# A sparse-attention plus feed-forward kernel: the first queries in a transfer of their own, and half of three up groups of block 0 moved into the round ahead

## What is computed

```python
scores = scale * np.matmul(q, k.transpose(0, 1, 3, 2))
kth = np.partition(scores, -top_k, axis=-1)[..., -top_k:-top_k + 1]
scores = np.where(scores >= kth, scores, -1000000000.0)
...
x = attn_out.transpose(0, 2, 1, 3).reshape(2304, 512)
h = x @ w_in
g = h * np.tanh(np.where(h > 20.0, h, np.log1p(np.exp(np.minimum(h, 20.0)))))
y = g @ w_out
```

## Time and profile before

| | |
|---|---|
| median of three runs | 761.02 us |
| the profiled execution: its time | 761.13 us |
| its span, first to last instruction | 759.3 us |
| PE busy | 720.5 us (95%) |
| DVE busy | 700.5 us (92%) |
| ACT busy | 570.3 us (75%) |
| POOL busy | 494.3 us (65%) |

### The profile page before, as it was taken

How to read it: one execution, slowest core, us unless ns; L and a number is a source line. 1 busy time by engine, 2 the same in 40 slices (tenths; PEclk the granted TensorE clock), 3 DMA queues, 4 the chain that set the end, 5 groups by cost and what they waited for, 6 DMA issues and landing times.

```text
span 759.3 us, 16003 instructions
## 1 busy us (share of the span) xinstructions
PE 720.5 (95%) x6056; PEld 625.3 (82%) x6056; DVE 700.5 (92%) x1512; ACT 570.3 (75%) x942; POOL 494.3 (65%) x590
## 2 busy tenths in 40 slices
PE   4258999999999999999999999999999999999998
PEld 2147888888989898979898989898888888888987
DVE  5999999999999999999999999999999999999600
ACT  3576978787879787878787777878796969687831
POOL 1877858576766666666667585848585858585813
PEclk9998999999999999999999999999999999999999
DMA  7560000031230000111110000001122000000000
GB/s 273 179 214 14 8 22 8 22 104 57 66 102 9 12 20 8 40 33 38 47 52 8 23 8 22 9 22 43 57 78 91 6 22 8 22 2 15 1 15 15
DMA packets 22684, 34.06 MB, mean 45 GB/s; under 512 B 2384, under 2 KB 11600, under 8 KB 22096
## 3 DMA queue, kind: packets, MB, share of 16 engines
q1 hardware_dynamic: 22608, 33.04, 13.3%
HBM read 28.31 MB, written 4.72 MB: 43 GB/s over the span
## 4 chain that ended last, share of the span: by engine, by line
PE 92%; DVE 6%; DMA 0%; issue 0%; ACT 0%; POOL 0%; SPq 0%
PE ps_u L397 35%; PE ps_y L412 27%; PE ps_o L379 10%; PE ps_s L351 9%; PE ps_s L332 9%; DVE left L601 3%; DVE top L607 2%; PE ps_o L372 1%; PE ps_s L328 1%; DVE top L592 1%; DMA q_sb<-q_in 0%; POOL p_sb L674 0%; ACT x_sb L459 0%; ACT xT L499 0%; ACT y_sb L528 0%
## 5 line engine op out<-in xcount | busy, mean ns | idle before, releaser
L607 DVE MAX8 top<-left 128x8 f32<-128x576 f32 x432 | 304.8, 747 | 0.0
L397 PEld LDWEIGHTS ps_u<-xT,win 128*128 128x128 f32 x2304 | 262.5, 192 | 13.8 <-issue 11.1
L397 PE MATMUL ps_u<-xT,win 128*128 128x128 f32 x2304 | 271.8, 277 | 0.7 <-ACT xT L499 0.7
L601 DVE MATCH_REPLACE8 left<-top,left 128x576 f32<-128x576 f32 x288 | 211.8, 743 | 0.0
L659 POOL TENSOR_TENSOR p_sb<-x_sb,p_sb 128x576 f32<-128x576 f32 x144 | 202.4, 1422 | 8.5 <-ACT p_sb L469 8.4
L489 ACT ACTIVATE pT<-ps_s 128x512 f32<-128x512 f32 (+1 forms) x144 | 85.6, 646 | 71.1 <-PE ps_s L351 71.1
L478 ACT ACTIVATE p_sb<-p_sb,neg_max 128x576 f32<-128x576 f32 x144 | 110.6, 769 | 27.7 <-POOL p_sb L659 27.2
L674 POOL TENSOR_SCALAR p_sb<-p_sb,recip 128x576 f32<-128x576 f32 x144 | 106.2, 747 | 35.6 <-DVE recip L582 35.6
L412 PE MATMUL ps_y<-w_hi,g_hi 128*128 128x512 f32 x288 | 117.9, 409 | 0.0
L469 ACT ACTIVATE p_sb<-x_sb,limit 128x576 f32<-128x576 f32 x144 | 105.5, 772 | 12.6 <-POOL limit L649 12.5
L412 PE MATMUL ps_y<-w_hi,g_lo 128*128 128x512 f32 x288 | 112.5, 391 | 0.0
(11 more groups left out here) (30 smaller groups left out, 603.5 us busy)
## 6 DMA issues: line engine op xcount, KB each, us to landing
v_sb<-v_in SPq DMA_DIRECT2D x32, 320.0 KB, 3.5
k_sb<-k_in SPq DMA_DIRECT2D x16, 288.0 KB, 3.3
q_sb<-q_in SPq DMA_DIRECT2D x68, 64.0 KB, 1.8
g_raw<-w_out SPq DMA_DIRECT2D x8, 512.0 KB, 4.4
win<-w_in SPq DMA_DIRECT2D x4, 1024.0 KB, 8.9
y_out<-y_sb SPq DMA_DIRECT2D x16, 256.0 KB, 2.0
y_out<-y_sb SPq DMA_DIRECT2D x4, 128.0 KB, 2.3
q_sb<-q_in SPq DMA_DIRECT2D x1, 256.0 KB, 3.4
```

The costliest lines, as they stand in the source:

```text
L397: mm = pe.matmul(ps_u[:, n % 2, i, :], win[:, k, P * f:P * f + P], xT[:, k, :], start=(k == 0), stop=(k == KC - 1), skip_group_check=True)
L601: dve.match_replace(out=left[:, t, :], in_to_replace=best[:, t, EIGHT * r:EIGHT * r + EIGHT], in_values=x[t] if r == 0 else left[:, t, :], ...
L607: dve.max(best[:, t, EIGHT * r + EIGHT:EIGHT * r + 2 * EIGHT], left[:, t, :]).then_inc(found, 1)
```

## The change

The queries of duo 0 get a transfer of their own (64 KB) ahead of the keys of pair 0; those of duos 1 to 3 follow behind the keys. `copy_xT(0)` is cut in two: `copy_xT_early` copies the pairs 0 and 1 of `ps_o` as soon as `values(1)` is through, in the round of -1, and `copy_xT(0)` the other two. On PE `up_begin(j)` runs the eight matmuls with k = 0 and 1 of the groups j = 0, 1 and 2 in the round of -1, and `up(0, j)` the eight with k = 2 and 3. Group 2 stands in the bank of `ps_y` for this block. The four loads of `w_in` have a semaphore each.

```diff
+EARLY, BEGUN = 2, 3
...
-                sp.dma_start(win[:, k, :], w_in[P * k:P * k + P, :]).then_inc(win_loaded, 16)
+                sp.dma_start(win[:, k, :], w_in[P * k:P * k + P, :]).then_inc(win_loaded[k], 16)
...
+            sp.dma_start(q_sb[:, 0, :], q_in[0, :, :]).then_inc(q_loaded[0], 16)
             load_k(0)
-            sp.dma_start(q_sb[:, :, :], q_in[0:QS, :, :].rearrange("s p c -> p s c")).then_inc(q_first, 16)
+            sp.dma_start(q_sb[:, 1:QS, :], q_in[1:QS, :, :].rearrange("s p c -> p s c")).then_inc(q_first, 16)
...
             def values(s):
...
+                if s == 2:
+                    pe.wait_ge(xT_begun, 1)
...
+            def up_bank(m, j):
+                if m == 0 and j == 2:
+                    return ps_y[:, :].rearrange("p (i c) -> p i c", i=FPG)
+                return ps_u[:, (GROUPS * m + j) % 2, :, :]
+
+            def up_begin(j):
+                if j == 0:
+                    pe.wait_ge(win_loaded[0], 16)
+                    pe.wait_ge(win_loaded[1], 16)
+                    pe.wait_ge(xT_begun, 1)
+                for i in range(FPG):
+                    f = FPG * j + i
+                    for k in range(EARLY):
+                        pe.matmul(up_bank(0, j)[:, i, :], win[:, k, P * f:P * f + P], xT[:, k, :],
+                                  start=(i == 0 and k == 0), stop=False, skip_group_check=True)
...
             def up(m, j):
...
-                if n >= 2:
+                if n >= 3:
                     pe.wait_ge(up_copied, n - 1)
+                begun = m == 0 and j < BEGUN
...
-                    for k in range(KC):
+                    for k in range(EARLY if begun else 0, KC):
...
             def down(m, j):
...
                 if m == 0 and j == 0:
                     pe.wait_ge(wlo_ready, WCHUNKS)
+                    pe.wait_ge(up_copied, BEGUN)
...
                 values(4 * m + 4)
                 values(4 * m + 5)
+                if m == -1:
+                    up_begin(0)
+                    up_begin(1)
                 down(m, 0)
                 transposes(4 * m + 6)
                 down(m, 1)
                 scores(4 * m + 10)
+                if m == -1:
+                    up_begin(2)
                 down(m, 2)
                 down(m, 3)
                 transposes(4 * m + 7)
...
+            def copy_xT_early():
+                act.wait_ge(out_ready, EARLY)
+                act.activation(xT[:, 0:EARLY, :], ps_o[:, 0:EARLY, :], ACT.Copy).then_inc(xT_begun, 1)
...
-                act.activation(xT[:, :, :], ps_o[:, :, :], ACT.Copy).then_inc(xT_copied, 1)
+                pairs = slice(EARLY if m == 0 else 0, PPB)
+                act.activation(xT[:, pairs, :], ps_o[:, pairs, :], ACT.Copy).then_inc(xT_copied, 1)
...
                 exp(4 * m + 6, 1)
+                if m == -1:
+                    copy_xT_early()
                 copy_up(m, 3)
                 copy_x(4 * m + 9, 0)
```

More of the change, by code:

```diff
@@ L158, in program @@
         v_loaded = [sem(f"v_loaded{i}") for i in range(PPB)]
-        win_loaded = sem("win_loaded")
+        win_loaded = [sem(f"win_loaded{i}") for i in range(KC)]
+        xT_begun = sem("xT_begun")
         wout_loaded = [sem(f"wout_loaded{i}") for i in range(2)]
@@ L309, in scores @@
                     pe.wait_ge(k_loaded[g % (KS * PPB)], 16 * (g // (KS * PPB)) + 16)
-                if s == 0:
+                if s == 1:
                     pe.wait_ge(q_first, 16)
+                elif s % QS == 0:
+                    pe.wait_ge(q_loaded[0], 16 * (s // QS) + 16)
                 elif s >= QS:
@@ L388, in up @@
                 if n == 0:
-                    pe.wait_ge(win_loaded, 16 * KC)
+                    for k in range(EARLY, KC):
+                        pe.wait_ge(win_loaded[k], 16)
                 if j == 0:
                     pe.wait_ge(xT_copied, m + 1)
-                if n >= 2:
+                if n >= 3:
                     pe.wait_ge(up_copied, n - 1)
+                begun = m == 0 and j < BEGUN
                 for i in range(FPG):
                     f = FPG * j + i
-                    for k in range(KC):
-                        mm = pe.matmul(ps_u[:, n % 2, i, :], win[:, k, P * f:P * f + P], xT[:, k, :],
+                    for k in range(EARLY if begun else 0, KC):
+                        mm = pe.matmul(up_bank(m, j)[:, i, :], win[:, k, P * f:P * f + P], xT[:, k, :],
                                        start=(k == 0), stop=(k == KC - 1), skip_group_check=True)
@@ L511, in copy_up @@
                     act.wait_ge(glo_ready, 2 * (m - 1) + j // 2 + 1)
-                act.activation(g_raw[:, FPG * j:FPG * j + FPG, :], ps_u[:, n % 2, :, :],
-                               ACT.Copy).then_inc(up_copied, 1)
+                bank = ps_y[:, :].rearrange("p (i c) -> p i c", i=FPG) if n == 2 else ps_u[:, n % 2, :, :]
+                act.activation(g_raw[:, FPG * j:FPG * j + FPG, :], bank, ACT.Copy).then_inc(up_copied, 1)
             def mish(m, h):
```

## The result

The changed kernel takes 765.02 us (median of ten runs, 762.0 to 766.32) against 761.49 us of the kernel before (ten runs, 760.89 to 762.31): the ratio is 1.0041, 95% interval 1.0027 to 1.0054. It is slower by 0.4%.

What follows compares the result with a forecast made beforehand. PE was taken as saturated behind 59.24 us, but held to DVE's equally saturated pace up to `transposes(5)`. +2.3 (DVE's wait) - 0.1 (removed work) - 0.3 (first transfer) = +1.9 us on 761.13 gave 763.0, median 762.9; range 760.5 to 766.3 us.

Steps and rivals of the forecast that it cites:

- The likeliest case, 762.9 us: The forecast: DVE waits and the clock stays; own range 762.2 to 763.6 us, chance 0.44.
- the clock case: Rival: PE's clock also falls to half ahead of `transposes(5)`, costing 1.8 to 3.4 us; 764.7 to 766.3 us, chance 0.33.
- 0.34 + 0.33: Chance of slower by over 0.2%: 0.34 of the forecast's 0.44 plus all of the clock case, given as 0.66.
- 0.10 us to win at `transposes(5)`: DVE's `normalise(5)` bounds `transposes(5)`, so of 5.5 us taken off PE only 0.10 us can show.
- DVE waits at `inverse(3)`: Late `transposes(2)` delays the chain through ACT and POOL to `inverse(3)`; DVE waits 4.2 - 1.9 = 2.3 us.
- The 4.2 us from `values(1)` to `transposes(2)`: Delay of `transposes(2)`: 0.5 us round trip for the early copy plus 3.67 us for sixteen matmuls.
- The first transfer, 0.3 us: At the start, keys issued second land at about 4.27 us, so PE and DVE begin 0.3 us earlier.
- The gap ahead of `transposes(5)`: PE, free at 77.3 us, would sit idle for 3.6 us until `transposes(5)` at 80.95 us.
- DVE is not made to wait: Rival: `transposes(2)` less than 1.9 us later, so `inverse(3)` has no wait; 760.6 us, chance 0.18.
- the chain's slack (1.9 us here): Time between `guard(3)` ending and DVE running `inverse(3)`: 57.38 - 55.43 - 0.05 = 1.9 us.

Runs made afterwards that it cites:

- e12: Changed kernel with the begun groups behind `scores(6)` and twelve discarded matmuls in PE's gap ahead of `transposes(5)`: 760.72 us, ratio 0.9991.
- e10: Kernel before with 24 discarded matmuls in PE's gap ahead of `transposes(3)`, behind `scores(6)`: 760.96 us, ratio 0.9995.
- e6: Kernel before with sixteen discarded matmuls added between `values(1)` and `transposes(2)`, nothing taken away: 763.60 us, ratio 1.0023.
- e3: Changed kernel with the three begun groups behind `scores(6)` and the early copy behind `penalty(3, 0)`: 762.39 us, ratio 1.0012.
- e1: Kernel before with the transfer edit alone (queries of duo 0 first): 761.36 against 761.76 us, ratio 0.9995.
- e4: Changed kernel with twelve discarded matmuls in PE's idle stretch ahead of `transposes(5)`: 762.70 us, ratio 1.0015.
- e9: Changed kernel with begun groups behind `scores(6)` and two of four column blocks of `up(0, 3)` ahead of `transposes(5)`: 760.28 us, ratio 0.9985.
- e5: Changed kernel with `up(0, 3)` moved ahead of `transposes(5)`: 762.52 us, ratio 1.0012.

## Why the prediction was right or wrong

The range of 760.5 to 766.3 us held the time, and slower was the likeliest outcome. The likeliest case, 762.9 us, was not what most runs did. The median of 765.02 us lies in the clock case, 764.7 to 766.3 us: the range held it because it took in a rival of chance 0.33, not because the forecast was near. Two slips of arithmetic: the forecast's own terms give about 762.5 to 763.5 us and not 762.2 to 763.6, and 0.34 + 0.33 is 0.67, not 0.66.

- **0.10 us to win at `transposes(5)`.** Right, and the base of the rest. The removal of 5.5 us, together with the earlier queries, is worth 0.24 us (e12 against e10), and `transposes(5)` moves no more than DVE's start does.
- **DVE waits at `inverse(3)`.** Right in place and links; e6 shows it without any removal, e3 shows it gone. I said 2.3 us; the profiles with the three begun groups in place show 1.3 to 2.5, as the clock rises earlier or later in `values(0)` and `values(1)`. In the profile at hand `values(1)` ended 1.3 us earlier than in that of before, and the wait is 1.0 us smaller. The 4.2 us from `values(1)` to `transposes(2)` were 53.12 - 48.89 = 4.23.
- **The first transfer, 0.3 us.** Right in mechanism: landing at 4.27 us was computed, and the scores start at 4.32. By the medians e1 can't tell it from nothing.
- **The gap ahead of `transposes(5)`.** I had 3.6 us; it is 3.59. It lies 1.2 us earlier than I had it, mostly because DVE's wait is 1.0 us smaller.
- **The clock.** This is the step that failed: the chance, not the mechanism. I gave the fall 0.33, on the ground that work is denser ahead of this gap than ahead of the one of before. By their mean clocks it came in 13 of 20 runs of the changed kernel, and a fourteenth is as slow. Its price, put at 1.8 to 3.4 us, measured 1.7 to 2.9 us in e3; between the two groups of the changed kernel lie 2.1 us or more, in which DVE's wait can have a part. The profiled 762.08 us and e3's 2.9 us make 765.0, the measured median. The rule of the Trainium skill's page "TensorE: Matmul & The Clock Gate" ("Why this matters for your kernels"), to leave PE no long idle gap between bursts, would have made this rival the forecast. e3 (3.59 us of idle, and by their mean clocks a fall in ten of eleven runs) and e4 (none behind 0.91 us in its profile) agree with it; the two profiles of the changed kernel show that the same gap can also pass without a fall.
- **DVE is not made to wait.** That rival fell. In the changed kernel no run is under 761.98 us.

## What to carry to other kernels

When two engines run at nearly the same pace, take the slack of the *other* engine at each hand-over before you count work taken off the first: here 5.5 us off the bound engine and an earlier first transfer together gained 0.24 us, and the earlier start accounts for all of it. Work that is filled into a gap should stand behind what a chain through other engines waits for; ahead of it, it makes the other saturated engine wait as soon as the chain's slack (1.9 us here) is used up. And idle time on TensorE that looks free can be paid for later at half clock, so compare runs with their granted clocks: with the gap filled by matmuls whose result is thrown away the changed kernel was 2.3 us faster.

## What the runs showed of the hardware

- A kernel of 761 us can be measured to 0.3 us or only to 3 us, as its idle gaps on TensorE let the clock fall or not, and as work hangs on the moment of the clock's first rise: e12 spreads over 0.31 us in eleven runs, the changed kernel over 4.3 us in ten, and e6, with the same mean clock in all its ten runs, over 3.1 us.
- The clock had not fallen in the 3.59 us of idle itself in e3's profile, but went to half as PE had resumed, and stayed there over saturated work. A gap of 1.80 us (e9) and one of 0.91 us (e12) left it alone in all eleven runs of each, whose mean clocks are 0.999 or 1.0.
- The length of the gap alone did not decide. In the profile of the changed kernel the clock stayed at 1.00 behind 3.59 us of idle ahead of `transposes(5)`, and fell to 0.50 behind 2.19 us of idle ahead of `transposes(3)`. In e5's profile 2.18 us of idle in that second place passed without a fall.
- In the kernels' first 50 us the granted clock is shown as 1.00, but a `transposes` at 30 or 40 us takes 2.15 to 2.18 us, and 1.15 to 1.20 later at a clock of 1.00. The lengths tell that TensorE ran at half clock up to 47 to 50 us. The trace's first record of the clock comes only then (at 47.2 us in the changed kernel, 49.2 in the kernel before), so a mean clock of 1.0 says nothing of that stretch.
